# Chaining the Strassen products of the up stage in PSUM, attention units every 14 steps, and the last batch's w_ch2 work spread out

## The reference, cut to what matters

```python
kv = einsum('bhsd,bhse->bhde', k, v); out = einsum('bhsd,bhde->bhse', q, kv)   # 8 batches, 8 heads, 576 x 64
x = out / sqrt(mean(out*out) + 1e-6) * g_norm                                  # heads joined: 8 x 576 x 512
u = x + (x^T @ U @ V)^T                                                        # low rank over the sequence
x2 = u + maximum(u @ w_ch1, 0) @ w_ch2                                         # 512 -> 2048 -> 512
# then a gated block: gelu(x2 @ w_in), layer norm, w_sg over the sequence, @ w_out, + x2
```

## Time and profile before

| | us |
|---|---|
| median of 3 runs | 1354.85 (1354.66 to 1355.14) |
| the profiled execution, its own time | 1356.87 |
| its span (first to last instruction) | 1355.1 |
| PE busy in the span | 1291.8 (95%) |
| DVE busy | 915.2 (68%) |
| ACT busy | 521.4 (38%) |
| mean granted clock of PE | 0.993 of full |

### The profile page before, as it was taken

How to read it: one execution, slowest core, us unless ns; L and a number is a source line. 1 busy time by engine, 2 the same in 40 slices (tenths; PEclk the granted TensorE clock), 3 DMA queues, 4 the chain that set the end, 5 groups by cost and what they waited for, 6 DMA issues and landing times.

```text
span 1355.1 us, 22351 instructions
## 1 busy us (share of the span) xinstructions
PE 1291.8 (95%) x8446; PEld 1238.0 (91%) x8446; DVE 915.2 (68%) x1300; ACT 521.4 (38%) x856; POOL 97.3 (7%) x107
## 2 busy tenths in 40 slices
PE   5789999999999998989999999999999999999998
PEld 5788999999999997989999999998898998988987
DVE  4977575656565659788889888895646446447443
ACT  4654434444443432545444454554312222222121
POOL 6220000000000000000000000000210111102100
PEclk9899999999999999999999999999999999999999
DMA  9444445454545425738346183634241350340421
GB/s 232 131 141 132 149 132 156 134 158 143 157 147 159 133 104 194 256 116 277 129 150 215 64 272 108 220 94 156 32 117 36 78 116 24 88 110 22 97 55 39
DMA packets 253831, 178.66 MB, mean 132 GB/s; under 512 B 165920, under 2 KB 224304, under 8 KB 253760
## 3 DMA queue, kind: packets, MB, share of 16 engines
q1 hardware_dynamic: 250800, 172.81, 42.8%
q0 software_dynamic: 1600, 4.56, 1.2%
q10 hardware_dynamic: 1360, 0.30, 0.1%
HBM read 109.47 MB, written 66.06 MB: 130 GB/s over the span
## 4 chain that ended last, share of the span: by engine, by line
PE 61%; issue 23%; DVE 8%; POOL 3%; ACT 3%; DMA 1%; SPq 1%; POOLq 0%; DVEq 0%; ACTq 0%
PE ps L1413 17%; PE ps L1415 17%; PE ps L1414 17%; PE ps L1434 2%; PE ps L1418 2%; PE ps L1442 2%; POOL rs L667 1%; POOL x_lo L661 1%; PE ps L1450 1%; DVE w L1031 1%; DVE h_st L1082 1%; ACT w L738 1%; PE ps L1461 1%; DVE y L998 1%; ACT y_hl L721 1%
## 5 line engine op out<-in xcount | busy, mean ns | idle before, releaser
L1413 PE MATMUL ps<-x_hi,w 128*128 128x288 f32 x896 | 273.0, 305 | 25.7 <-DVE h_st L1082 7.9
L1414 PE MATMUL ps<-x_lo,w 128*128 128x288 f32 x896 | 265.5, 296 | 0.0
L1415 PE MATMUL ps<-x_hi,w 128*128 128x288 f32 x896 | 265.1, 296 | 0.0
L1413 PE MATMUL ps<-r_hi,w_hi 128*128 128x384 f32 x672 | 225.0, 335 | 3.7 <-DVE r_lo L1210 2.7
L1414 PE MATMUL ps<-r_lo,w_hi 128*128 128x384 f32 x672 | 224.5, 334 | 0.0
L1415 PE MATMUL ps<-r_hi,w_lo 128*128 128x384 f32 x672 | 224.5, 334 | 0.0
L863 ACT ACTIVATE r_hi<-hb 128x768 fp32r<-128x768 f32 x168 | 142.2, 848 | 169.3 <-PE ps L1415 164.4
L1413 PEld LDWEIGHTS ps<-x_hi,w 128*128 128x128 f32 x896 | 169.6, 189 | 31.7 <-DVE h_st L1084 7.9
L1414 PEld LDWEIGHTS ps<-x_lo,w 128*128 128x128 f32 x896 | 169.8, 190 | 0.0
L1415 PEld LDWEIGHTS ps<-x_hi,w 128*128 128x128 f32 x896 | 169.8, 189 | 0.0
L1210 DVE TENSOR_TENSOR r_lo<-hb,r_hi 128x768 fp32r<-128x768 f32 x120 | 114.4, 956 | 34.5 <-ACT r_hi L863 34.5
(11 more groups left out here) (163 smaller groups left out, 2517.1 us busy)
## 6 DMA issues: line engine op xcount, KB each, us to landing
hT_scratch<-h_st SPq DMA_DIRECT2D x64, 576.0 KB, 4.6
hb<-hT_scratch SPq DMA_DIRECT2D x24, 1536.0 KB, 7.3
uT_scratch<-x_raw SPq DMA_DIRECT2D x32, 288.0 KB, 2.3
x_st<-uT_scratch SPq DMA_DIRECT2D x24, 384.0 KB, 3.7
x2T_scratch<-x_st SPq DMA_DIRECT2D x24, 384.0 KB, 6.9
x_raw<-x2T_scratch SPq DMA_DIRECT2D x8, 1152.0 KB, 5.8
xt_in<-x2T_scratch SPq DMA_DIRECT2D x144, 64.0 KB, 2.6
k_raw<-in_k SPq DMA_DIRECT2D x64, 128.0 KB, 3.0
```

The source lines that it names most:

```text
L1413: mm(dst, ws[0], xs[0], start=first, stop=False)
L1414: mm(dst, ws[0], xs[1], start=False, stop=False)
L1415: return mm(dst, ws[1], xs[0], start=False, stop=last)
```

## The change

Products are chained in PSUM. Product 2 is accumulated on product 0, product 4 on that, product 6 on that, and product 5 on product 1; only products 0, 1 and 3 begin an accumulation. A group uses three bank pairs, in two alternating assignments (`PAIR`). ACT makes four copies a group (products 0, 1, 2 and 6), DVE three sums (products 3, 4 and 5); the two sums within `h_st` are gone. An attention unit has a period of 14 steps, as long as a group: `QK` 2, `LOW` 7, `UT` 10, and `attention` of the next unit at 13 (`ATT`). The parts of the next tile's input and of w1, w_ch2 and h are placed at other steps, and SP issues `store_h` earlier at the passage to the last tile and at that to the down stage.

```diff
-BANK = (0, 1, 2, 0, 2, 0, 1)
-NADD = 7
+PAIR = ((0, 1, 0, 2, 0, 1, 0), (2, 1, 2, 0, 2, 1, 2))
+NADD = 3
+NCPY = 4
-PERIOD, QK, LOW, UT = 12, 2, 8, 11
+PERIOD, QK, LOW, UT, ATT = 2 * NI, 2, 7, 10, 13
...
             up_steps(B - 1, 0)
+            store_h(B - 2, NG - 1)
             load_w2(w2_raw[0], 0, 0, 0)
             load_w2(w2_raw[4], 1, 0, 1)
             load_w2(w2_raw[5], 2, 1, 1)
-            store_h(B - 2, NG - 1)
             load_w2(w2_raw[6], 3, 1, 0)
...
             load_hb(0, 3)
+            store_h(B - 1, NG - 1)
             load_w2(w2_raw[3], 4, 1, 0)
             sp.wait_ge(s_hst[0], 32 * 2 * B)
             load_u(0, C11)
             load_u(0, C22)
-            store_h(B - 1, NG - 1)
...
-                nc.scalar.activation(h_st[:, g % 2, :, 3 * idx, :], ps[:, 2 * BANK[idx]:2 * BANK[idx] + 2, 0:SH], ACT.Copy).then_inc(s_cp, 1)
+                o = 2 * PAIR[g % 2][idx]
+                nc.scalar.activation(h_st[:, g % 2, :, {0: 0, 1: 3, 2: 1, 6: 2}[idx], :], ps[:, o:o + 2, 0:SH], ACT.Copy).then_inc(s_cp, 1)
...
-            X_HIGH_AT = (HALF_UT + 2, HALF_UT + 4, LAST_UT + 4, LAST_UT + 5, LAST_UT + 8)
+            X_HIGH_AT = (26, 34, 53)
+            X_HIGH_THEN = (1, 2, 3, 6)
...
-                if idx == 2:
-                    dve.wait_ge(s_cp, 2 * n + 1)
-                    nc.vector.tensor_tensor(c12, p, c11, ALU.add).then_inc(s_ad, 1)
-                elif idx == 3:
-                    nc.vector.tensor_tensor(c11, p, c11, ALU.add).then_inc(s_ad, 1)
-                elif idx == 4:
-                    dve.wait_ge(s_ad, NADD * n + 1)
-                    nc.vector.tensor_tensor(c21, p, c12, ALU.add).then_inc(s_ad, 1)
-                    dve.wait_ge(s_cp, 2 * n + 2)
-                    nc.vector.tensor_tensor(c12, c12, c22, ALU.add).then_inc(s_ad, 1)
-                    dve.wait_ge(s_ad, NADD * n + 3)
-                    nc.vector.tensor_tensor(c22, c21, c22, ALU.add).then_inc(s_ad, 1)
-                elif idx == 5:
-                    dve.wait_ge(s_ad, NADD * n + 4)
-                    nc.vector.tensor_tensor(c12, p, c12, ALU.add).then_inc(s_ad, 1)
-                else:
-                    nc.vector.tensor_tensor(c21, p, c21, ALU.add).then_inc(s_ad, 1)
+                dve.wait_ge(s_cp, NCPY * n + idx - 2)
+                nc.vector.tensor_tensor(c, ps[:, o:o + 2, 0:SH], c, ALU.add).then_inc(s_ad, 1)
...
-                    if k in (14, 15, 16, 18):
-                        w2_sum((14, 15, 16, 18).index(k))
-                    if k in (20, 22, 32):
-                        w2_low((20, 22, 32).index(k))
+                    if k in (11, 13, 15, 17):
+                        w2_sum((11, 13, 15, 17).index(k))
+                    if k in (24, 26, 38):
+                        w2_low((24, 26, 38).index(k))
...
+                    if idx == 0 and not start:
+                        pe.wait_ge(s_ad, NADD * (n - 1) + 1)
+                    elif idx == 1 and not start:
+                        pe.wait_ge(s_ad, NADD * n)
+                    elif idx == 2:
+                        pe.wait_ge(s_cp, NCPY * n + 1)
+                    elif idx == 3 and not start:
+                        pe.wait_ge(s_cp, NCPY * n)
+                    elif idx == 4:
+                        pe.wait_ge(s_cp, NCPY * n + 3)
+                    elif idx == 5:
+                        pe.wait_ge(s_cp, NCPY * n + 2)
+                    elif idx == 6:
+                        pe.wait_ge(s_ad, NADD * n + 2)
```

More of the change, by code:

```diff
@@ L427, in up_tile @@
                 store_u(t + 1, 1)
+                store_h(t, 1)
                 load_next(m + 4)
[L429 removed]
                 store_u(t + 1, 2)
+                store_h(t, 2)
                 load_next(m + 5)
[L432 removed]
                 store_u(t + 1, 3)
@@ L804, in up_tile @@
                     g, idx, s_ = step(k)
[L805 to L810, removed]
                     r, at_ = hook(k)
@@ L813, in up_tile @@
                     more = r + 1 < HP or not end
-                    if at_ == 0:
+                    if at_ == QK + 1:
+                        y_high(m)
+                    if idx in (0, 1, 2, 6) and s_ == 1:
+                        copied(t, k)
+                    if first and k == 0:
                         attn_copy(m, BX, BY)
                         squares(m, sq)
-                    elif at_ == QK:
+                    if at_ == QK:
                         std(m)
@@ L830, in up_tile @@
                         u_evacuated(m, r, BX, 1 - par, t)
+                    elif at_ == ATT and more:
+                        attn_copy(m + 1, BX, BY)
+                        squares(m + 1, sq)
+                    if first and g + 1 < NG and at_ in (LOW, LOW + 2):
+                        w1_high(2 * g + (2, 3)[at_ == LOW + 2])
+                    if k in X_HIGH_THEN and not first:
+                        x_high(t, par, 3 + X_HIGH_THEN.index(k))
                     if k in X_HIGH_AT:
@@ L1120, in up_tile @@
                     g, idx, s_ = step(k)
-                    if idx > 1 and s_ == 1:
+                    if idx in (3, 4, 5) and s_ == 1:
                         added(t, k)
[L1123 to L1126, removed]
                     r, at_ = hook(k)
                     m = HP * (t + 1) + r
-                    if at_ == 2:
+                    if at_ == 1:
                         sums(m, sq)
-                    elif at_ == 3:
+                    elif at_ == 2:
                         normalise(m)
@@ L1134, in up_tile @@
                         y_low(m)
-                    elif at_ == LOW:
+                    elif at_ == LOW + 1:
                         a_split(m, BX)
-                    if k == HALF_UT + 1:
-                        x_sum(t + 1, 1 - par, 1)
[L1139 to L1142, removed]
-                    if k == LAST_UT + 3:
-                        x_sum(t + 1, 1 - par, 6)
-                    if k == LAST_UT + 4:
-                        x_low(t + 1, 1 - par, 1)
-                    if k == LAST_UT + 6:
-                        x_sum(t + 1, 1 - par, 4)
-                        x_low(t + 1, 1 - par, 2)
-                x_low(t + 1, 1 - par, 3)
+                    if k in X_LOW_THEN[2 if first else 0:]:
+                        x_low(t, par, 2 + X_LOW_THEN.index(k))
+                    if first and g + 1 < NG and at_ in (LOW + 3, LOW + 5):
+                        w1_low(2 * g + (2, 3)[at_ == LOW + 5])
+                    if k == 26:
+                        x_sum(t + 1, 1 - par, 1)
+                    if k in (33, 53):
+                        x_low(t + 1, 1 - par, (33, 53).index(k))
+                    if k in (52, 54, 55):
+                        x_sum(t + 1, 1 - par, {52: 2, 54: 6, 55: 4}[k])
             up_tile(0, 0, first=True)
@@ L1409, in _, with product @@
             mm = nc.tensor.matmul
-            def product(dst, ws, xs, first, last):
-                mm(dst, ws[0], xs[0], start=first, stop=False)
-                mm(dst, ws[0], xs[1], start=False, stop=False)
-                return mm(dst, ws[1], xs[0], start=False, stop=last)
+            def product(dst, ws, xs, first, last, chained=False):
+                mm(dst, ws[0], xs[0], start=first, stop=False, skip_group_check=chained)
+                mm(dst, ws[0], xs[1], start=False, stop=False, skip_group_check=chained)
+                return mm(dst, ws[1], xs[0], start=False, stop=last, skip_group_check=chained)
             def transpose(dst, src, start, stop=False):
@@ L1488, in _, with attention_step @@
             u_transposed(3, 4, y_first[0])
-            def attention_step(k, t, end):
+            def attention_step(k, t, first, end):
                 r, at_ = hook(k)
@@ L1495, in attention_step @@
                 more = r + 1 < HP or not end
-                if at_ == 0:
+                if first and k == 0:
                     pe.wait_ge(s_uev, m)
                     attention(m, BX, BY)
-                elif at_ == QK and more:
+                if at_ == QK and more:
                     pe.wait_ge(s_o, 2 * (m + 1))
@@ L1511, in attention_step @@
                     u_transposed(m, BX)
+                elif at_ == ATT and more:
+                    pe.wait_ge(s_uev, m + 1)
+                    attention(m + 1, BX, BY)
             def up_step(k, t, par, first):
@@ L1518, in up_step @@
                 start = first and g == 0
+                if first and idx == 0:
+                    pe.wait_ge(s_w1lo, a + 1)
                 if s_ == 0:
@@ L1544, in up_tile @@
                     if not final:
-                        attention_step(k, t, end)
+                        attention_step(k, t, first, end)
             up_tile(0, 0, first=True)
```

62 lines of the change are left out of this document (25 added, 37 removed).

## The result

| | before | after |
|---|---|---|
| median | 1354.99 (4 runs, 1354.66 to 1355.64) | 1322.61 (4 runs, 1320.52 to 1324.38) |
| the profiled execution, its own time | 1356.87 | 1322.69 |
| its span | 1355.1 | 1320.8 |
| DVE busy | 915.2 | 831.5 |
| ACT busy | 521.4 | 566.5 |

The ratio is 0.976, with a 95% interval of 0.9743 to 0.9777: 32 us faster, where 33.6 were forecast (a median of 1321.3). Part of the agreement is chance: the last tile came out longer, where it was to be shorter, and three other terms made up for it.

The account below looks back on a forecast made before the run. PE sets the pace, so only its waits can be won: 21.0 + 1.1 + 7.0 + 2.0 + 2.5 = 33.6 us, taken off the median of 1354.85, gives 1321.3 us. Forecast range 1317 to 1326 (chance 0.58); with A and B, 1311 to 1336.

Parts of the forecast that it names:

- middle tiles (2nd to 7th), the seventh's 1.1 with them: Up-stage tiles: PE's waits of 3.0 us a tile all go, and 1.1 more in the seventh.
- first tile, with its share of the 3.0: First up tile: 7.0 of 9.0 us of waits for `w1_low` and `a_split` won, besides the regular 3.0.
- last tile: Last up tile: 2.0 of 8.8 us won; a wait of 5.6 at product 6 stays, 1.2 for later groups.
- first down tile: Start of the down stage: the store is issued before the loads, so 2.5 us of PE's wait go.
- the rest of the span: Everything outside the up tiles and first down tile: not touched, PE-bound as before, no gain.
- 61.7 to 62: Sign in the profile after: middle tiles this many us long, without PE waits on `h_st`.
- The 2.0 kept for `a_split`: First tile: 2.0 us of waits left standing, as `a_split` on DVE is held up by POOL's sums.
- the forecast's own sign of being wrong: A last tile longer than before, or a regular wait on ACT's `h_st` at product 4 in every unit.
- A: Last and first tile: loads land in time, POOL is out of the way; some 8 us more, 1313; chance 0.14.
- B: Units: ACT's copy of product 2 comes late; +14 us (1335), or +7 (1328) at tile starts only; chance 0.20.
- C: Chained bank pairs: PE pays 1.02 us at three places of 32 groups, 1419 us; chance 0.06.
- D: Down stage: all that is won returns as waits on w_ch2, so no change; chance 0.02.

Follow-up runs that it names:

- pool_late: Changed kernel with POOL's w1 sums started at step 11 instead of step 4 of the first and second unit: 1323.97 us, ratio 0.9763.
- loads_first: Changed kernel with SP issuing the three w_ch2 loads before the store of the seventh tile's last group: 1318.00 us, ratio 0.9714.
- store_back: Changed kernel with the store of the last group put behind the loads of the down stage again: 1326.68 us, ratio 0.9780.
- the copies: Changed kernel with ACT's copy of product 2 made two, three or five times: 1325.06, 1332.60 and 1372.82 us.
- loads_first_sum4_late: The kernel of loads_first with the fourth w_ch2 sum also moved from step 17 to step 27: 1318.51 us, ratio 0.9720.

## Why the prediction was right, step by step

| step | predicted | measured |
|---|---|---|
| middle tiles (2nd to 7th), the seventh's 1.1 with them | -19.1 | -20.35 |
| first tile, with its share of the 3.0 | -10.0 | -9.77 |
| last tile | -2.0 | +1.41 |
| first down tile | -2.5 | -4.32 |
| the rest of the span | 0 | -1.3 |
| sum of the span | -33.6 | -34.3 |

The spans differ by more than the medians (32.4), as the profiled execution of before lay 1.9 above its median and that of after 0.1.

**Middle tiles.** The step held: PE was the pace, its waits were all there was to win, and all of them went. The size was 3.3 a tile, not 3.0, as a tile of 61.44 leaves 16.6 beside its steps, and 16.9 were reckoned; 61.7 to 62 had been named as the sign. The seventh won 5.47 where 4.1 were reckoned. 1.1 of that is no gain but work: one of its attentions now runs in the first tile, which the forecast, with its equal count of matmuls, had overlooked. Against these, the loop's jump took 1.8 back in the third tile (-1.54 in place of -3.3), because the wait that had covered it was gone; nothing in the forecast held a price for the loop.

**First tile.** It won 9.77 where 10.0 were forecast, but made up otherwise. The 2.0 kept for `a_split` were too many: POOL still holds its operations (1.41 for 0.28, as in the earlier trace rows), yet PE loses only 0.34 + 0.17 = 0.5 by it. In their place 0.8 went for `w`, and 1.1 for the fifth attention, which the forecast lacks. These and the opening make up 6.0 of the 6.2 by which the tile is longer than a middle one: its step 8 starts 13.40 us in (58.67), where the middle tile's does after 8.71, and of these 4.7 us 1.1 are the attention and 3.6 the slow start that the forecast had at 3.65. The two ends of the moved attention cancel in the sum; as neither was in the forecast, that is luck. That the removed sums would free POOL was seen: one of its sums takes 1.29 where the same one took 3.07 before. The Trainium skill's rule (SBUF — State Buffer, Who interferes with whom), that an operation of DVE with two SBUF inputs and a reading GpSimd shut each other out, agrees with these rows in both directions (POOL 3.07 to 1.29, `w1_low` 2.02 to 3.12 in `pool_late`). The under 1 us that the forecast drew from it was nearer to the measured 0.5 than the 2.0 taken from the rows.

**Last tile.** This is the step that failed, and by the forecast's own sign of being wrong, a last tile that is longer than before (54.98 for 53.57). The forecast had a wait of 5.6 on product 6 of the second group, at the right place and for the right reason (the first sum, for which the third load was reckoned at 16, starts 17.3 into the tile), and 1.2 for the rest. Measured are 6.68 + 0.17 for the wait, 2.1 for the three steps at half clock behind it, and 0.92 for the wait at 534.51, with small change some 10.2 against 6.8. So the wait came out 1.2 longer, and the sum had no term for the low clock behind it: before the change the wait of 4.12 was followed by a window from 534 to 538 at a granted clock of 0.64, which was there to be read. `loads_first` shows what the order cost, 54.98 less 50.37.

**Down stage.** The cause was right, as `store_back` shows, and the term too small, 4.32 for 2.5. It priced only the wait behind the copy. Before, PE lost another 0.53, 0.47 and 0.79 at three places 26 to 32 us into the tile; these went too, and came back with the store in `store_back` (0.52, 0.47, 0.82), so they were the store's as well; one new loss, of 0.69, stands 28 us into the tile.

**The rivals.** A (the edges go too) did not come by itself; half of it had to be made with `loads_first`. B and C are refuted by the middle tiles, in which PE never waits, and by the copies: 0.69 to spare and no wait at one copy more. D is refuted by the rest of the span, which did not grow.

Two things stay open: why the same stop of PE is followed by half clock in some executions and not in others, and how the rest of the span won its 1.3 us (0.4 ahead of the first tile, 0.9 behind the first down tile).

## What to carry to other kernels

Read each wait against the margin of the next reader in the queue. When regular waits go, what they covered (here the loop's jump) becomes the price, and the way to know a margin is to lengthen its operation until the wait shows. When one queue carries a store and a load that are both wanted first, one of them is late; decide by what it holds up. Count behind a wait of PE also the slow matmuls that may follow it, and before a gain or loss of 1 to 2 us is put down to an edit, look whether the two traces had the same clock there: the later fourth sum looked like a gain of 1.5 us and was none. When work is moved, count it on both sides of every boundary that is measured. Moving an operation away from a neighbour that slows it is worth only what its next neighbour doesn't lose.

## What the runs showed of the hardware

- A jump back of PE's loop cost 2.35 us, shown in the profile as a wait for data that had long been there.
- After a wait of 6.68 us PE worked 4.5 us at 1.2 GHz (granted 0.50, 0.25 a matmul where 0.133 is usual) before it was back at 2.4 GHz.
- Shorter stops were followed by such a stretch in some executions only, and it began about 1 us after PE had restarted. A wait on ACT of 2.6 us was followed by it in `loads_first` (1.5 us lost) and not in `loads_first_sum4_late`; the stop at the loop's jump was followed by it in the latter and in `store_back` (1.5 us), and not in the changed kernel.
- SP's issues took longer the more was ahead of them in its queue: four loads of 1 MB behind a store took 7.58 us, where the three of the earlier trace rows had taken 2.38 and the one store 1.18 (in `loads_first`, behind three loads, a store took 3.75):

```profile
482.36 1.18 SPq L384 DMA_DIRECT2D hT_scratch<-h_st  x2
483.58 7.58 SPq L389 DMA_DIRECT2D w_raw<-in_moe_w_ch  x4
```

- Accumulating onto a bank that was read out in between cost PE nothing that can be seen: a middle tile with four chained products a group runs at the pace of its matmuls, 61.4 busy of 61.4.
